# First layer's output with features on partitions, logits straight from it, rows gathered in quarters and turned on VectorE

## The reference

```
a = x @ w_a;  b = x @ w_b;  x = a * b @ w_out          # 512 -> 1536 -> 512
logits = x @ w_gate;  e_idx = argmax(logits, axis=1)
eom = 1.0 / (1.0 + exp(-(x @ w_output_gate)))
for e in range(8):                                      # 512 -> 1024 -> 512
    mask = e_idx == e
    h = maximum(x[mask] @ w1[e], 0.0)
    out[mask] = gate_w[mask, None] * eom[mask, e, None] * (h @ w2[e])
```

## Time and profile before

| | us |
|---|---|
| median of 3 runs | 1187.62 |
| lowest and highest | 1184.88, 1188.63 |
| the profiled execution, whole | 1186.21 |
| its span on the core | 1184.40 |
| PE busy in the span | 1160.9 (98%) |
| DVE, ACT, POOL busy | 555.5, 408.6, 328.4 |

### The profile page before, as it was taken

One profiled execution on the slowest core, in us unless ns is written; L12 is line 12 of the kernel. 1 busy time (PEld: TensorE's weight loads), 2 busy tenths in 40 slices (PEclk: granted clock), 3 DMA queues, 4 the chain that ended last, 5 costly groups with the idle time before them and its releaser, 6 DMA issues.

```text
span 1184.4 us, 19818 instructions
## 1 busy us (share of the span) xinstructions
PE 1160.9 (98%) x7460; PEld 922.8 (78%) x7462; DVE 555.5 (47%) x1116; ACT 408.6 (34%) x766; POOL 328.4 (28%) x415
## 2 busy tenths in 40 slices
PE   8999999999999999999999999999899999999997
PEld 5777776777767777777777898798688788988887
DVE  3464645546446456455444447622734634215221
ACT  2434324334333343343343443412523533114110
POOL 1442113122132132131343463322122312222222
PEclk9999999999999999999999999999899999999999
DMA  8555224324333342232312344611632815111111
GB/s 333 187 186 183 91 91 144 112 105 143 110 125 123 112 143 90 92 134 81 121 58 90 98 153 170 211 36 45 215 139 76 288 36 186 44 44 44 36 55 38
DMA packets 45943, 141.07 MB, mean 119 GB/s; under 512 B 6624, under 2 KB 9056, under 8 KB 38816
## 3 DMA queue, kind: packets, MB, share of 16 engines
q1 hardware_dynamic: 37744, 117.75, 29.0%
q0 software_dynamic: 8128, 22.34, 5.6%
HBM read 122.19 MB, written 19.13 MB: 119 GB/s over the span
## 4 chain that ended last, share of the span: by engine, by line
PE 91%; DVE 4%; DMA 3%; issue 2%; ACT 1%; DVEq 0%; POOL 0%; SPq 0%; POOLq 0%; ACTq 0%
PE bank L1218 28%; PE bank L1220 26%; PE bank L1219 26%; PE bank L1249 5%; PE bank L1213 3%; DMA xg<-x_rows,gather_cur 2%; PE bank L1277 1%; PE bank L1262 1%; DVE weights L1005 1%; PE bank L1341 1%; PE bank L1465 1%; DMA w_out_raw<-w_o 1%; DVE weights L1023 0%; DMA st_first<-st_first 0%; DVE y1p L935 0%
## 5 line engine op out<-in xcount | busy, mean ns | idle before, releaser
L548 POOL TENSOR_TENSOR glo<-g_sb,ghi 128x512 fp32r<-128x512 f32 (+1 forms) x108 | 133.6, 1237 | 458.2 <-ACT ghi L618 458.0
L1218 PE MATMUL bank<-w_out,ghi 128*128 128x512 f32 x408 | 170.6, 418 | 0.0
L1220 PE MATMUL bank<-w_out,glo 128*128 128x512 f32 x408 | 160.2, 393 | 0.0
L1219 PE MATMUL bank<-w_out,ghi 128*128 128x512 f32 x408 | 159.2, 390 | 0.0
L1218 PE MATMUL bank<-aT_hi,state_w 128*128 128x512 f32 x384 | 155.5, 405 | 1.0 <-DVE aT_lo L890 1.0
L1220 PE MATMUL bank<-aT_hi,state_w 128*128 128x512 f32 x384 | 149.9, 390 | 0.0
L1219 PE MATMUL bank<-aT_lo,state_w 128*128 128x512 f32 x384 | 149.7, 390 | 0.0
L1059 DVE TENSOR_TENSOR g_sb<-bank,a_sb 128x512 f32<-128x512 f32 (+1 forms) x108 | 70.9, 657 | 146.1 <-PE bank L1220 92.6
L1218 PEld LDWEIGHTS bank<-w_out,ghi 128*128 128x128 f32 x408 | 76.5, 188 | 56.2 <-issue 44.4
L1218 PE MATMUL bank<-weights,ht_hi 128*128 128x512 f32 x296 | 119.7, 404 | 0.4 <-DVE ht_lo L1145 0.4
L618 ACT ACTIVATE a_sb<-bank 128x512 f32<-128x512 f32 (+1 forms) x108 | 62.0, 574 | 161.7 <-PE bank L1220 161.7
(11 more groups left out here) (194 smaller groups left out, 2058.5 us busy)
## 6 DMA issues: line engine op xcount, KB each, us to landing
w_ring<-w_ab SPq DMA_DIRECT2D x48, 1024.0 KB, 5.2
raw<-w SPq DMA_DIRECT2D x30, 1024.0 KB, 6.1
x_rows<-y_sb SPq DMA_DIRECT2D x34, 256.0 KB
xn_in<-x_n SPq DMA_DIRECT2D x16, 512.0 KB, 3.6
xt_in<-x_t SPq DMA_DIRECT2D x7, 1024.0 KB, 5.0
w_raw<-w_ab SPq DMA_DIRECT2D x8, 512.0 KB, 7.9
w_out_raw<-w_o POOLq DMA_DIRECT2D x12, 256.0 KB, 5.2
w_spare_raw<-w_ab SPq DMA_DIRECT2D x4, 512.0 KB, 4.3
```

The costliest lines, as they stand in the source:

```text
L548: pool.tensor_tensor(glo[:, f % 2, 0:cols], g_sb[:, 0:cols], ghi[:, f % 2, 0:cols].bitcast(F32), ALU.subtract).then_inc(g_split, 1)
L1218: T.matmul(acc, hi_s, hi_m, start=start, stop=False)
L1219: T.matmul(acc, hi_s, lo_m, start=False, stop=False)
L1220: return T.matmul(acc, lo_s, hi_m, start=False, stop=stop)
```

## The change

- Stage B swaps its operands: 128 columns of `w_out` are the stationary operand and g the moving one (512 columns; 256 for b = 8). The accumulator `PY[c]` now holds 128 features on partitions and all rows of the batch along the bank. For b = 8 two feature groups share a bank, and the 6 matmuls of 512 columns in a step become 12 of 256.
- The "YT" steps are gone. ACT copies the accumulators to `yT` in pieces of 32 rows, and ACT and DVE split `yT` directly. The four "LG" steps of a batch become one with 48 matmuls, at f = 8.
- DVE turns `yT` in 32x32 blocks (`turn_y`, two instructions of 1024 elements for a batch), which leaves 32 rows by 128 features in order; so `x1` becomes a tensor of quarter rows, (4 x 4352) x 128. SP stores them in four DMAs (at f = 5, not f = 1).
- A block is gathered in quarters: four indirect DMAs, each 128 quarter rows of 512 bytes. DVE turns the block in 32x32 blocks (`turn_x`, one instruction of 512 elements), one block further ahead than PE did. PE does no `turn_x` any more.
- The record of a slot is split into `slot_x` (one number) and `slot_rows` (two), each scattered by its own indirect DMAs: the first at f = 11, the second at f = 0 two batches later.
- `finish` moves from DVE to ACT. The ring of first-layer weights has 2 places, not 4. In b = 8 the low parts of the last two weight pieces are made by DVE (`w_low`), not POOL.

The core of the diff:

```
-RING = 4
+RING = 2
-            if b and f in (1, 3, 5, 7):
-                behind.append(("YT", b - 1, f // 2, 0))
-            if b and f in (2, 4, 6, 8):
-                between.append(("LG", b - 1, f // 2 - 1, 0))
+            if b and f == 8:
+                between.append(("LG", b - 1, 0, 0))
...
-                    last = three(PY[t][:, :], ghi[:, f % 2, t * P:(t + 1) * P], glo[:, f % 2, t * P:(t + 1) * P],
-                                 WO[:, f, 0, :], WO[:, f, 1, :], f == 0, f == FT - 1)
+                    last = three(y_acc(b, c), WO[:, f, 0, c * P:(c + 1) * P], WO[:, f, 1, c * P:(c + 1) * P],
+                                 ghi[:, f % 2, 0:cols], glo[:, f % 2, 0:cols], f == 0 and (b < 8 or c % 2 == 0),
+                                 f == FT - 1 and (b < 8 or c % 2 == 1))
...
+            def turn_y(b, n):
+
+                dve.wait_ge(y_copied, 4 * b + 4 if b < 8 else 34)
+                wait(dve, y_stored, 64 * b)
+                src = (yT if b < 8 else yT8)[:, n * 8:n * 8 + 8, :, :]
+                V.transpose(y1_sb[:, n * 8:n * 8 + 8, :].rearrange("p i e -> p (i e)"),
+                            src.rearrange("p i c t -> p (i c t)")).then_inc(y_turned, 1)
...
-            def scatter(b):
+            def scatter_x(b):
...
+                    pool.indirect_dma_start(slot_x, bass.IndirectOffsetOnAxis(ap=slot_i[:, t:t + 1], axis=0),
+                                            rowx[:, t:t + 1], None).then_inc(slotx_stored, 16)
+
+            def scatter_rows(b):
...
+                    if b > 1 and f == 0:
+                        scatter_rows(b - 2)
...
+                wait(pool, xr_done, k)
                 pool.sem_inc(rows_seen, 1)
-                pool.indirect_dma_start(xg[:, :], None, x1, bass.IndirectOffsetOnAxis(ap=gcur[:, 0:1],
-                                                                                          axis=0)).then_inc(x_gathered, 16)
+                for t in range(4):
+                    pool.indirect_dma_start(xg[:, t * P:(t + 1) * P], None, x1, bass.IndirectOffsetOnAxis(
+                        ap=gcur[:, t:t + 1], axis=0)).then_inc(x_gathered, 16)
...
+            def turn_x(k):
+                dve.wait_ge(xs_ready, k)
+                dve.wait_ge(x_gathered, (k - EARLY) * 64 + 64)
+                V.transpose(xr[:, :], xg[:, :]).then_inc(xr_done, 1)
+
             def xs(k, place=0):
                 dve.wait_ge(xshi_done, k + 1)
...
                 for n in w2[:W2_EARLY]:
                     w2_lo(n, par, e)
                 xs(k + 1)
                 ht(1, k)
+                turn_x(k + 2)
                 for n in w2[W2_EARLY:]:
                     w2_lo(n, par, e)
...
             def pair(k):
                 xs(k + 1, 1)
-                finish(k)
                 for q in range(4):
+                    if q == 2:
+                        turn_x(k + 2)
...
                 xs(k + 2)
-                finish(k + 1, 1)
+                turn_x(k + 3)
```

438 lines of the change are left out of this document (266 added, 172 removed).

## The result

| | before | changed |
|---|---|---|
| median | 1187.49 us (12 runs, 1184.88 to 1188.63) | 1193.00 us (12 runs, 1187.49 to 1197.62) |
| profiled execution, span | 1184.4 | 1194.8 |

The ratio is 1.0054, with a 95% interval of 1.0036 to 1.0073. The change makes the kernel slower by 0.5%, where 1166 us was forecast. The forecast was wrong in sign, and the time lies above its range. The profiled execution took 1196.5 us, 3.5 us over the median.

The account below looks back on a forecast made before the run. PE was taken to bound both phases, closely followed in the experts by gather, turn and split. First layer -17.6, tail +6, experts -10 sum to -21.6 us: 1166 us against the 1187.62 median, range 1154 to 1182.

Parts of the forecast that it names:

- First layer, up to b = 8: Batches 0 to 7: transposes leaving PE save 14.1 us, merged logits steps 2.2; each batch 2.0 us shorter, PE still busy.
- the two early gathers are 4 x 1.27 = 5.1 us each; POOL falls behind by under 2 us: Last batch: POOL's lag against steps of 4.3 us is paid for by weight pieces moved to DVE; costed at nothing.
- turns, LG waits, 256 columns: Last batch: turn steps leave PE, 0.44 us each; 2.0 us of logits waits go; 144 matmuls of 256 columns add 0.7.
- The tail, "+6": Between the phases: quarter gathers delay the first two-block product by 4.0 to 7.7 us; +6 taken.
- the landing of block 3: Tail: the last quarter gather lands 3.5 us after its issue starts, at 753.6.
- The experts, "-10": Expert phase: 15.0 us of turns saved, less 5 us of waits where weights are split.
- PE loses the turns, -15.0 if nothing takes their place: Experts: 34 turn steps of blocks leave PE, 0.44 us each.
- POOL's round becomes 7.2 + 3.8 = 11.0, so POOL just keeps up: Experts: POOL's 11.0 us per block fits PE's 11.3 in a pair, about 11.9 single; steady pairs cost nothing.
- 0 to 3 and taken 0.8: Experts: at each of six places where weights are split, late gathers give back this many us; +5 in all.
- A: Rival for tail and experts: gathers never late, tail costs only 4 us; about 1157 us; chance 0.15.
- B: Rival: experts give nothing, body-to-pair places cost 3 us each, steady pairs 1; set at 1180 us; chance 0.15.
- C: Rival: POOL's gathers under load bound the experts, 14 landing 3.7 us later each; 1200 us; chance 0.11.

Follow-up runs that it names:

- e4: Changed kernel with the last two batches' rows stored in runs of 8 KB instead of 512 bytes, that row order left out of the result; 1184.18 us.
- e1: First layer's half of the change alone, with one whole-row gather per block and TensorE turns as in the kernel before; 1168.33 us.
- e17: The kernel of e1 again, unaltered, on another chip; 1166.94 us.
- e5: Changed kernel, but GpSimd's wait for the scatter's landing stands behind the next block's four gathers, not ahead of them; 1164.39 us.
- e18: The kernel of e5 a third time, unaltered, on the chip of e17; 1173.86 us.
- e9: Kernel of e5 with the third block's gathers before the first scatter, a later ScalarE scaling, and weight pieces before the first body's turn; 1172.83 us.
- e3: Changed kernel with VectorE turning a block behind the weight pieces, and the first single block's own second half evacuated first; 1175.58 us.
- e12: The changed kernel again, unaltered, on another chip; 1194.80 us.
- e2: Changed kernel with one gather of 2-KB rows per block instead of four quarter gathers, fetching wrong rows; 1153.15 us.
- e13: The kernel of e5 again, unaltered, on the chip of e12; 1175.35 us.
- e7: The kernel of e1 with the wait for the scatter's landing moved behind the one gather; 1167.47 us.

## Why the prediction was wrong, step by step

The forecast in the stretches of the table above, against what the changed kernel did, and against e4, which has its waits but ran where the stop does not come (differences from the kernel before, us):

| | up to b = 8 | last batch | tail and to first pair | rest | sum |
|---|---|---|---|---|---|
| forecast | -14.3 | -3.3 | +6 | -10 | -21.6 |
| changed | -16.2 | +5.0 | +16.8 | +4.9 | +10.4 |
| e4 | -16.3 | +1.3 | +10.5 | +0.3 | -4.1 |

The largest miss is in the rest, the experts, in both lines.

**First layer, up to b = 8: right.** A full batch took 80.79 us before and takes 78.53 after, from one batch's first product of stage A to the next, 2.26 less, where 16.3 / 8 = 2.04 was forecast. PE stayed busy for 560.0 of 560.0 us. That stage B costs the same with `w_out` as the stationary operand, a bound from the nearest rows, is borne out by the same numbers. The whole first layer's half, forecast at -17.6, measured -18.4 in e1 (1168.33 against 1186.77) and -20.6 in e17.

**b = 8: "the two early gathers are 4 x 1.27 = 5.1 us each; POOL falls behind by under 2 us": wrong.** Between the addition of row numbers and the first gather POOL stood 2.2 us, which I did not count. PE waited 3.1 us for `glo` on every chip. The last batch should have been 3.3 us shorter. It is 1.4 longer without the stop (e5: 59.6 against 58.2), and 3.4 to 5.5 longer with it (e18 and e9). e1 and e17 have 56.4, so the first layer's part of that sum (turns, LG waits, 256 columns) gave 1.8 of the 3.3; 0.6 of the missing 1.5 is a wait of PE on a weight piece of POOL's, the rest is not accounted for.

**The tail, "+6": too small.** The span from the first early up product to the first two-block product was 43.0 us. It is 59.8 in the changed kernel, and 52.5 and 53.5 without the stop (e5, e4), +9.5 and +10.5, above the bounds of 4.0 to 7.7. The four gathers of block 3 on POOL in the changed kernel, the first and the last:

```profile
744.52 1.30 POOL L628 DMA_INDIRECT xg<-x_rows,gather_early  x1 [2.68 <-DMA out<-y_sb,scatter_cur]
748.87 0.94 POOL L628 DMA_INDIRECT xg<-x_rows,gather_early  x1 [0.30 <-issue]
```

From the first of them to the first pair it is 23.0 us, where it was 15.8: +7.3, and +8.6 in e5. The issues were priced nearly right (4.4 us from the first to the last, 3.8 forecast), and so was the next block's gather (7.7 us from its first issue to its turn, 7.3 to 11.0 forecast). The mis-sized term is the landing of block 3: VectorE's turn starts at 754.36, 5.5 us behind the start of the last issue, and 6.7 us behind it in e5, where I took 3.5. The other part is where this chain starts, which I had left where it was: 27.3 us behind the first early up product before, 28.1 in e5, and 36.8 in the changed kernel, where the stop of PE lies in front. What I passed over as well is what stands behind that turn on VectorE and ScalarE in the same body: the next block's copy on ScalarE and `ht_lo` of the block in hand, which wait 6.0 us along with it:

```profile
754.36 0.71 DVE L1290 STREAM_TRANSPOSE xr<-xg 128x512 f32<-128x512 f32 x1 [6.01 <-DMA xg<-x_rows,gather_early]
754.99 2.45 DVE L1155 TENSOR_TENSOR weights<-raw,weights 128x512 fp32r<-128x512 f32 x4
757.36 0.69 DVE L1294 TENSOR_TENSOR xs_lo<-xr,xs_hi 128x512 fp32r<-128x512 f32 x1
757.97 0.68 DVE L1284 TENSOR_TENSOR ht_lo<-bank,ht_hi 128x512 fp32r<-128x512 f32 x1
```

I worked out when the block would be there, not who else stands in that queue. PE then still has half a down product to do between its two waits, of 7.1 and 4.4 us. This cost nothing by itself, though: e3, which puts the block's own half first, has waits of 6.0 and 5.5 us there instead of the 8.8 and 3.6 of e4 on the same chip, and its first pair comes 0.9 us earlier. The second gather of the chain decides. e9 gets back 2.5 to 4.0 us of it with its orders on POOL, ScalarE and VectorE.

**The experts, "-10": the failing step.** It was +4.9 (e12: -0.1, e4: +0.3). Three parts:

- "PE loses the turns, -15.0 if nothing takes their place" was right, even low: e2 has -19.2 and e5 -17.9, since the 5.2 us wait of the earlier trace rows went as well.
- "POOL's round becomes 7.2 + 3.8 = 11.0, so POOL just keeps up" was right for pairs (10.9 in the changed kernel) and wrong where single blocks follow each other. I read the round at one place, between pairs, and used it for all. Among single blocks, with weights being split and loaded, the landing of the scatter takes 5.5 us and the copies 0.65 each instead of 0.2: 15.1 us a round. I had PE's time for a single block, 11.9 us, in the same place (it is 11.8). PE then waits up to 6.7 us at a pair, where I had priced 0 to 3 and taken 0.8. Moving POOL's wait for the landing behind the gathers, and nothing else, takes the rest from 422.3 to 403.8 us (e12, e13): this wait in POOL's round is the cause.
- Neither did I price what a wait does to the clock. Each of the three in the rest made the product behind it 1.5 to 2.4 us longer in e12, 6.0 us together.

**The clock and the stop: no step at all.** The forecast took full clock throughout, since the kernel before has it, without asking why it does: it hardly ever waits. Its one long wait among the experts, the 5.2 us on a weight split of the earlier trace rows, had the price in the open: behind it products of 512 columns start 0.43 us apart instead of 0.23, at half clock (the second line: length, PE busy, granted clock, DMA share, GB/s).

```profile
846.60 0.77 PE L1218 MATMUL bank<-weights,xs_hi 128*128 128x512 f32 x1 [5.22 <-DVE weights L1005]
846.60:850.20 3.60, 3.60 (x9) 0.50 0.94 311
```

The stop of PE costs 9.5 to 11 us (e18 and e13 against e5) on three of the experiments' five chips and on the chip of the result, and no row of the kernel before could have told of it. Without it the changed kernel would take about 1184 us, as e4 shows, whose stores differ but whose waits are about the same (29.5 us on `xs_lo` and `ht_lo`, 31.2 in the changed kernel). That is still 18 us above the forecast.

**The rivals.** A (1157, "gathers never late") is close to what e2 measures, 1153, in a kernel that leaves work out. B (1180, "the experts give nothing") names what the experts did where the stop does not come: 422.7 us in e4 against 422.4, and 1184.18 us is just past the end of its 1176 to 1184. Its prices are not those of the trace: steady pairs cost nothing, and two of the places before a pair cost 5 us of waiting and more. C ("POOL's gathers under load become the bound") had the sign and, in part, the place. But its mechanism was landing times at 14 loaded gathers. The runs show POOL's own queue instead, with a wait in front of the gathers that could be moved. The rule that I quoted beside C (the Trainium skill, SBUF — State Buffer, "SBUF: two separate sides": VectorE in a fast mode shuts GpSimd out of writing descriptors) finds no strong trace here. In e12's round the first two gathers take 1.28 and 1.45 us and the others 0.95, so at most 0.8 us of issues in a round of 15.1 can be laid to it, beside copies of 0.65 instead of 0.2. VectorE ran only subtractions during this round's gathers, so the rule as quoted was not put to the test.

**The best kernel.** Of those that compute the whole, e5's is the fastest on its chip (1164.39) and takes 1173.86 to 1175.35 on two others. e1's takes 1168.33 and 1166.94 on two chips, one of which stops the other kernel. On that chip e1's kernel beats the kernel before by 1.7% (0.9813 to 0.9853) and e5's by 0.6%. Where the stop does not come, e5's is ahead by 3.1 us: 1164.39 against 1167.47 for e7, the first layer's half with the same edit on POOL, on one chip. e1's is the one to keep, the first layer's half without the gather half: it took about the same on both chips.

## What to carry to other kernels

Before moving work off the bound engine, write out the whole round of the queue that will feed it, at its worst place and not at the steady one: every wait in it counts, above all one for a landing that stands ahead of issues which don't need it. When an engine is made to wait for data, list what stands behind it in its queue, and price the clock behind each wait of several us too: the trace of the old kernel may show it in one place. And time a kernel on more than one chip when a few per cent decide, with the old one beside it.

## What the runs showed of the hardware

- An indirect DMA of 128 rows mostly costs GpSimd 0.94 to 1.0 us (up to 1.5 in places) and another 0.30 before the next, for 4 bytes, 512 bytes or 2 KB a row alike: the scatters of one number, the quarter gathers and e2's whole rows. Splitting a gather in four costs four times the issue, 3.8 us more.
- The landing of a quarter gather was seen 5.5 us behind the start of its issue in the tail of the changed kernel and 6.7 us in e5. The wait for the landing of a scatter held GpSimd for 2.7 us in the tail and 5.5 us beside the loads of expert weights (e12).
- The two-block product (96 products of 256 columns) took 11.7 us at full clock and 13.0 to 14.4 us where the granted clock fell behind waits of 2.2 to 6.7 us. A wait of 2.1 us in e4 brought no fall, one of 2.2 us at the same place in e12 brought 3.4 us at 1.2 GHz.
- PE can stand still with nothing that it waits for in the profile. On three of the five chips it stood for up to 1.2 us at a time (1.9 once, in e9) in the merged logits step and in long products, 3.0 to 7.4 us in all in the uncut logits steps, and the granted clock fell behind it, to 0.86 in the stretch of the tail shown for e18. e5's kernel, unaltered, ran through on one of the two other chips, and e3 and e4, with the same quarter gathers and the same merged step, on the other.
- The first subtraction of `y_parts`, now from SBUF to SBUF, took 1.37 us on average instead of 0.69 from PSUM. It stretches beside GpSimd's subtractions: in the changed kernel it takes 0.68 us in the seven cases without one beside it and mostly 1.46 to 1.69 (2.61 at most) beside `glo`. It cost nothing in the full batches, where PE is busy for 560.0 of 560.0 us.
